# Softmax maxima and inverse sums spread by DMA, scores half a tile further ahead, one output bank per MLP, weight setup reordered

## The reference

```
kv_flat = mean over 4x4 windows of kv, @ w_sr        # 768 keys, k = v
s = (q @ k.T) / sqrt(128);  s = s - s.max(-1)
a = exp(s);  a /= a.sum(-1) + 1e-9;  x = a @ v
h = x @ w_in1;  y = (max(h, 0) + alpha * min(h, 0)) @ w_out1      # 2048 hidden features
h = y @ w_in2;  out = (h * sigmoid(1.702 h)) @ w_out2
```

## Time and profile before

| | us |
|---|---|
| median of 3 runs | 1409.24 (1408.22 to 1411.01) |
| span of the profiled execution | 1407.1 |
| TensorE busy | 1365.1 (97%) |
| VectorE busy | 1088.8 (77%) |
| ScalarE busy | 823.9 (59%) |
| GpSimd busy | 444.9 (32%) |

### The profile page before, as it was taken

One profiled execution on the slowest core, in us unless ns is written; L12 is line 12 of the kernel. 1 busy time (PEld: TensorE's weight loads), 2 busy tenths in 40 slices (PEclk: granted clock), 3 DMA queues, 4 the chain that ended last, 5 costly groups with the idle time before them and its releaser, 6 DMA issues.

```text
span 1407.1 us, 19487 instructions
## 1 busy us (share of the span) xinstructions
PE 1365.1 (97%) x6000; PEld 1094.6 (78%) x6000; DVE 1088.8 (77%) x1689; ACT 823.9 (59%) x1417; POOL 444.9 (32%) x295
## 2 busy tenths in 40 slices
PE   4599999999999999999999999999999999999998
PEld 3477887887887878878878788788787787887776
DVE  6868878778678787787786887877968877778775
ACT  2465665656656656656566566565665665655644
POOL 2740522413405314234054142241440522413400
PEclk8699999999999999999999999999999999999999
DMA  7100000000000000000000000000000000000000
GB/s 255 68 1 16 0 15 15 0 15 7 7 15 7 7 15 0 15 7 7 15 7 7 15 0 15 15 0 15 7 7 15 0 15 15 0 15 0 8 8 8
DMA packets 9514, 23.26 MB, mean 17 GB/s; under 512 B 1184, under 2 KB 1312, under 8 KB 8992
## 3 DMA queue, kind: packets, MB, share of 16 engines
q1 hardware_dynamic: 6048, 16.85, 3.6%
q10 hardware_dynamic: 3456, 6.29, 1.2%
HBM read 16.85 MB, written 6.29 MB: 16 GB/s over the span
## 4 chain that ended last, share of the span: by engine, by line
PE 90%; DVE 6%; ACT 1%; DMA 1%; issue 0%; SPq 0%; DVEq 0%; ACTq 0%
PE ps_y L639 14%; PE ps_y L641 13%; PE ps_y L640 13%; PE ps_h L641 12%; PE ps_h L639 12%; PE ps_h L640 12%; PE ps_s L639 4%; PE ps_s L640 4%; PE ps_s L641 4%; DVE g_lo L545 3%; PE ps_t L670 2%; PE ps_t L682 2%; DMA kv_raw<-kvT 1%; ACT g_full L372 1%; DVE g_hi L543 1%; DVE wide L502 0%
## 5 line engine op out<-in xcount | busy, mean ns | idle before, releaser
L283 POOL TENSOR_TENSOR s_sb<-s_sb,max_sb 128x512 f32<-128x512 f32 x138 | 205.3, 1523 | 577.6 <-ACT max_sb L349 577.6
L537 DVE SCALAR_TENSOR_TENSOR g_lo<-ps_h,g_hi 128x512 fp32r<-128x512 f32 x384 | 264.0, 688 | 153.1 <-ACT g_hi L367 150.5
L372 ACT ACTIVATE g_full<-ps_h 128x512 f32<-128x512 f32 x384 | 229.8, 598 | 252.6 <-PE ps_h L641 247.6
L545 DVE TENSOR_TENSOR g_lo<-g_full,g_hi 128x512 fp32r<-128x512 f32 x384 | 309.6, 806 | 13.1
L639 PE MATMUL ps_y<-g_hi,down_hi 128*128 128x512 f32 x768 | 313.4, 408 | 1.6 <-DVE g_lo L545 0.5
L641 PE MATMUL ps_y<-g_hi,down_lo 128*128 128x512 f32 x768 | 303.4, 395 | 0.0
L640 PE MATMUL ps_y<-g_lo,down_hi 128*128 128x512 f32 x768 | 302.4, 394 | 0.0
L367 ACT ACTIVATE g_hi<-ps_h 128x512 fp32r<-128x512 f32 x384 | 229.1, 597 | 94.2 <-PE ps_h L641 81.7
L543 DVE CAST g_hi<-g_full 128x512 fp32r<-128x512 f32 x384 | 161.9, 422 | 28.1 <-ACT g_full L372 28.0
L639 PEld LDWEIGHTS ps_y<-g_hi,down_hi 128*128 128x128 f32 x768 | 144.7, 188 | 47.7 <-DVE g_lo L545 18.6
L515 DVE TENSOR_TENSOR a_lo<-s_sb,a_hi 128x512 fp32r<-128x512 f32 x144 | 171.3, 1190 | 1.2 <-ACT a_hi L362 1.2
(11 more groups left out here) (90 smaller groups left out, 1774.9 us busy)
## 6 DMA issues: line engine op xcount, KB each, us to landing
kv_raw<-kvT SPq DMA_DIRECT2D x12, 512.0 KB, 5.4
q_raw<-qT SPq DMA_DIRECT2D x24, 256.0 KB, 2.6
outT<-out_sb ACTq DMA_DIRECT2D x24, 256.0 KB, 2.0
w_raw<-w_in SPq DMA_DIRECT2D x2, 1024.0 KB, 6.2
w_raw<-w_out SPq DMA_DIRECT2D x2, 1024.0 KB, 7.3
wsr_sb<-w_sr SPq DMA_DIRECT2D x1, 64.0 KB, 3.2
alpha_sb<-alpha SPq DMA_DIRECT2D x1, 8.0 KB, 3.5
```

What stands on the lines that cost most here:

```text
L283: nc.gpsimd.tensor_tensor(s_sb[:, c, :], s_sb[:, c, :], max_sb[:], ALU.subtract).then_inc(diff_done, 1)
L372: nc.scalar.activation(g_full[:, f % RING, :], ps_h[:, f % RING, :], ACT.Gelu_apprx_sigmoid).then_inc(act_done, 1)
L537: nc.vector.scalar_tensor_tensor(g_lo[:, f % RING, :], ps_h[:, f % RING, :], 0.0, f32(g_hi[:, f % RING, :]), ALU.max, ALU.subtract).then_i ...
L545: nc.vector.tensor_tensor(g_lo[:, f % RING, :], g_full[:, f % RING, :], f32(g_hi[:, f % RING, :]), ALU.subtract).then_inc(g_split, 1)
```

## The change

The maxima and the inverse sums no longer go through `wide`, four transposes and a PSUM bank. SP stores the 128x4 column to a row of 512 values in the chip's memory and loads that row back to all 128 partitions (`spread_max`, `spread_inverse`). The bank `ps_t` goes, and so does one bank of `ps_s`, which now takes scores and turned columns by turns; `ps_x` holds the attended values, which VectorE reads there directly; `ps_y1` and `ps_y2` hold the outputs of the two MLPs. Scores, maxima and queries now belong to tile t + 2: scores in the GELU half, queries in the relu half. Eight of the 16 GELU casts go to ScalarE, the output store goes from ScalarE to SP, and a tiny GELU loads ScalarE's table ahead of the copy of y. Ahead of the loop w_in1 comes already turned, the second MLP's weights have a place of their own and are split in pieces of 512 columns, and the scores of tile 1 are made there.

The diff, cut to its core (constants, banks, SP, GpSimd, ScalarE, VectorE, TensorE; `spread_inverse` is made as `spread_max`, and waits for the division before it instead of the subtraction):

```diff
+    EXP_AT = {7: 0, 9: 1, 10: 2, 12: 3, 13: 4, 15: 5}
+    LO_AT = {8: 0, 10: 1, 11: 2, 13: 3, 14: 4}
+    ATTEND_AT = {11: 0, 13: 1, 14: 2}
+    QUERIES_AT = 5
+    SUMS_AT = LAG
+    SCORES_AT = {5: 0, 7: 1, 8: 2, 10: 3, 12: 4, 13: 5}
+    DIVIDE_AT = 9
+    CAST_ON_ACT = (1, 3, 5, 7, 9, 11, 13, 15)
+    max_row = nc.dram_tensor("max_row", (BLOCKS, P), F32, kind="Internal").ap()
+    inv_row = nc.dram_tensor("inv_row", (BLOCKS, P), F32, kind="Internal").ap()
...
-        ps_s = psum("ps_s", [P, 2, 512])
-        ps_t = psum("ps_t", [P, 512])
-        ps_y = psum("ps_y", [P, 512])
+        ps_x = psum("ps_x", [P, 512])
+        ps_s = psum("ps_s", [P, 512])
+        ps_y1 = psum("ps_y1", [P, 512])
+        ps_y2 = psum("ps_y2", [P, 512])
...
+            def spread_max(u):
+                sp.wait_ge(col_max_done, u + 1)
+                with nc.allow_non_contiguous_dma(reason="a column of 512 values"):
+                    sp.dma_start(max_row.rearrange("b p -> p b"), col_max[:]).then_inc(max_stored, DMA)
+                if not first(u):
+                    sp.wait_ge(diff_done, u * KC)
+                sp.wait_ge(max_stored, u * DMA + DMA)
+                row = max_row.rearrange("b p -> (b p)").rearrange("(o n) -> o n", o=1)
+                sp.dma_start(max_sb[:], row.broadcast_to([P, TOK])).then_inc(max_in, DMA)
...
+            load_queries(1)
+            spread_max(0)
+            load_queries(2)
+            spread_inverse(0)
+            spread_max(1)
+            with sp.Fori(0, TILES - 3) as t:
+                load_queries(t + 3)
+                spread_inverse(t + 1)
+                spread_max(t + 2)
+                store(t)
...
-            with pool.Fori(1, TILES - 1) as u:
-                subtract_max(u)
-                sum_exponentials(u)
-                queries_lo(u + 1)
+            for m, (hi, lo) in enumerate(((up_hi[1], up_lo[1]), (down_hi[1], down_lo[1]))):
+                for i in range(PIECES):
+                    pool.wait_ge(w2_hi, m * PIECES + i + 1)
+                    nc.gpsimd.tensor_tensor(lo[:, piece(i)], w_raw2[:, m * FF + i * PIECE:m * FF + (i + 1) * PIECE],
+                                            f32(hi[:, piece(i)]), ALU.subtract).then_inc(w2_lo, 1)
+            with pool.Fori(0, TILES - 2) as t:
+                queries_lo(t + 2)
+                subtract_max(t + 1)
+                sum_exponentials(t + 1)
...
+                if f in CAST_ON_ACT:
+                    act.wait_ge(act_done, t * UPS + (CH + f + 1))
+                    nc.scalar.copy(g_hi[:, f % RING, :], g_full[:, f % RING, :]).then_inc(act_cast, 1)
...
+            def tile(t, attend, score):
                 for f in range(LAG, CH):
...
+                    relu_hi(t, f)
+                    if attend and f in EXP_AT:
                         exponentials(t + 1, EXP_AT[f])
...
                         exponentials_hi(t + 1, EXP_AT[f])
...
+                nc.scalar.activation(warm_out[:], warm[:], ACT.Gelu_apprx_sigmoid)
...
+                    if score and f in SCORES_AT:
+                        scores_to_sbuf(t + 2, SCORES_AT[f])
...
+            act.dma_start(w_in1T_sb, w_in1T).then_inc(w_in[2], DMA)
             scores_to_sbuf(0, KC - 1)
+            act.wait_ge(pooled_made, KV_CHUNKS)
+            act.dma_start(w_raw2[:, 0:FF], w_in2).then_inc(w_in[3], DMA)
+            act.dma_start(w_raw2[:, FF:2 * FF], w_out2).then_inc(w_in[4], DMA)
...
+            for c in range(KC):
+                scores_to_sbuf(1, c)
+            act.wait_ge(w_in[3], DMA)
+            for i in range(PIECES):
+                nc.scalar.copy(up_hi[1][:, piece(i)], w_raw2[:, i * PIECE:(i + 1) * PIECE]).then_inc(w2_hi, 1)
             attended_hi(0)
...
-                dve.wait_ge(x_raw_made, u + 1)
-                dve.wait_ge(inv_spread, u + 1)
-                nc.vector.tensor_tensor(x_full[:], x_full[:], ps_t[:], ALU.mult).then_inc(x_made, 1)
...
+            def tile(t, attend, score):
                 for f in range(LAG, CH):
...
                     relu_lo(t, f)
...
+                    if score and f == QUERIES_AT:
+                        queries_hi(t + 2)
+                    if attend and f in LO_AT:
+                        weights_lo(t + 1, LO_AT[f])
+                for c in range(len(LO_AT), KC if attend else 0):
+                    weights_lo(t + 1, c)
                 dve.wait_ge(y_hi_made, t + 1)
...
+                nc.vector.tensor_tensor(y_lo[:], ps_y1[:], f32(y_hi[:]), ALU.subtract).then_inc(y_split, 1)
                 for f in range(CH):
                     gelu_parts(t, f)
...
+                    if attend and f == SUMS_AT:
                         inverse_sums(t + 1)
...
+                    if score and SCORES_AT.get(f, 0) >= 1:
+                        chunk_max(t + 2, SCORES_AT[f])
+                    if attend and f == DIVIDE_AT - 1:
                         divide(t + 1)
...
+                    if attend and f == DIVIDE_AT:
                         attended_lo(t + 1)
...
+                if attend:
                     for f in range(LAG):
                         relu_lo(t + 1, f)
+                        if score and f == 1:
+                            token_max(t + 2)
...
+                elif c == 0:
+                    pe.wait_ge(col_sum_done, u)
+                else:
+                    pe.wait_ge(scores_out, u * KC + c)
...
+            def tile(t, attend_next, score):
                 for f in range(LAG, CH):
                     up(t, 0, f)
...
                     down(t, 0, f - LAG)
...
+                    if attend_next and f in ATTEND_AT:
                         attend(t + 1, ATTEND_AT[f])
...
+                passes(ps_y1[:], mix_hi[:], mix_lo[:], x_hi[:], x_lo[:], False, False)
                 for f in range(CH - LAG, CH):
                     down(t, 0, f)
...
+                for c in range(len(ATTEND_AT), KC if attend_next else 0):
+                    attend(t + 1, c)
+                if first(t):
+                    pe.wait_ge(w2_lo, 2 * PIECES)
                 for f in range(CH):
                     up(t, 1, f)
...
+                    if attend_next and f == SUMS_AT:
                         turn_sums(t + 1)
...
+                    if score and f in SCORES_AT:
+                        scores(t + 2, SCORES_AT[f])
                     if f >= LAG:
                         down(t, 1, f - LAG)
                 for f in range(LAG):
...
+                    if attend_next:
                         up(t + 1, 0, f)
+                        if score and f == 1:
+                            turn_max(t + 2)
                     down(t, 1, CH - LAG + f)
...
+            turn_sums(0)
+            for c in range(KC):
+                scores(1, c)
             pe.wait_ge(up0_lo_made, 1)
             for f in range(LAG):
                 up(0, 0, f)
+                if f == 1:
+                    turn_max(1)
```

More of the change, by code:

```diff
@@ L22 @@
 DMA = 16
+PIECE = 512
 def attention_mlp_kernel(
@@ L208, in cols, with piece, score_bank, casts_before @@
             return slice(b * P, (b + 1) * P)
+        def piece(i):
+            return slice(i * PIECE, (i + 1) * PIECE)
         def first(t):
             return isinstance(t, int) and t == 0
[L213 to L220, removed]
+        def score_bank(u, c):
+            return ps_x[:] if first(u) and c % 2 == 0 else ps_s[:]
+        mix_ps = ps_y1[:, 0:C]
+        CASTS_ACT = len(CAST_ON_ACT)
+        CASTS_DVE = CH - CASTS_ACT
+        def casts_before(f, on_act):
+            return sum((j in CAST_ON_ACT) == on_act for j in range(f))
         block = ctx.enter_context(nc.Block())
@@ L242, in _ @@
             sp.dma_start(w_raw[1][:], w_out1).then_inc(w_in[1], DMA)
[L244 to L258, removed]
+            load_queries(1)
[8 more added lines that the diff above has]
+                store(t)
+            spread_inverse(TILES - 2)
+            spread_max(TILES - 1)
+            store(TILES - 3)
+            spread_inverse(TILES - 1)
+            store(TILES - 2)
+            store(TILES - 1)
+            sp.wait_ge(out_stored, DMA * TILES)
         @block.gpsimd
@@ L575, in tile @@
                         inverse_sums(t + 1)
-                    if not last and f == SPREAD_SUMS_AT:
+                    if score and SCORES_AT.get(f, 0) >= 1:
+                        chunk_max(t + 2, SCORES_AT[f])
+                    if attend and f == DIVIDE_AT - 1:
                         divide(t + 1)
-                    if not last and f == SPREAD_SUMS_AT + 1:
+                    if attend and f == DIVIDE_AT:
                         attended_lo(t + 1)
-                    if prepare and f == CH // 2:
-                        queries_hi(t + 2)
@@ L582, in tile @@
-                if not last:
+                if attend:
                     for f in range(LAG):
                         relu_lo(t + 1, f)
+                        if score and f == 1:
+                            token_max(t + 2)
             per_chunk = KV_CHUNKS // KC
```

(15 more changed lines are left out.)

289 lines of the change are left out of this document (107 added, 182 removed).

## The result

The kernel after takes **1712.92 us** (median of 4 runs, 1710.02 to 1715.44) against 1408.95 of the kernel before, run beside it: ratio **1.2151, 95% interval 1.2133 to 1.217**. The prediction said 1381, within 1374 to 1403. The miss is 332 us.

The account below looks back on a forecast made before the run. TensorE, busy 97% of the span, was taken to bound the kernel. Terms -20.2 (transposes), -10.9 (gaps), -4.2 (scores leaving the loop), +5 (preamble) and +1 (small waits) gave -29 us: 1381 us, within 1374 to 1403.

Parts of the forecast that it names:

- the price of the trip: Column stored by SP and loaded as a row to 128 partitions: 5.4 us, of which store 2.6; maxima hidden up to 7.5.
- the late row: Rival: the row of maxima comes too late, costing 22 x (R - 7.5) for a trip of R us; chance 0.12.
- The second trip: Inverse sums in the GELU half: row at 9.3 us, division at about 11.5, about 3 us of room behind; costs nothing.
- the break-even: Before attend(0): GpSimd waits for the maxima past a 6.9 us trip; TensorE loses time one for one past 7.5 us.
- the tile: Steady tile of the loop: 54.4 to 54.6 us, against 55.84 before.
- a set of transposes: Four transposes on TensorE cost 0.44 us; removing two sets in each of 23 tiles gains 20.2 us.
- the table load that hides: ScalarE's 1.28 us load ends about 0.4 us before y is complete; rival that it does not hide: +12 us, chance 0.06.
- one bank: One bank for scores and turned sums adds no wait; rival of 0.3 us a tile, +7 us, chance 0.14.
- the maxima of tile 1 behind x_lo: At the start, the third up waits some 2 us for these maxima, giving an effective start of 76.5.
- The preamble: Ahead of the loop: first up at 74.5, loss of 5 us (bounds +2 and +9); rival +9 more, chance 0.08.
- the gaps: Two TensorE gaps a tile, 0.32 and 0.16 us, from slow VectorE subtractions beside GpSimd; ending both gains 10.9 us.

Follow-up runs that it names:

- the kernel with 16 byte runs: The kernel after, with each transpose taking every fourth token, so a store writes 128 runs of 16 bytes instead of 512 of 4: 1390.76 us, ratio 0.9865.
- one extra load: Against the 16 byte layout, SP loads the row of maxima once more to an unused place and waits for it before the load that counts: 1446.21 us.

## Why the prediction was wrong

**The step that failed** is the price of the trip, the 5.4 us that it was given. It was bounded by the two nearest rows, a 256 KB store and the small `alpha` load: 2.0 to 3.5 us for the store, 2.6 for the load. Neither row writes runs of four bytes, and the text said so ("no row prices 512 descriptors of 4 bytes"), yet it took the quiet end and gave the late row a chance of 0.12. The store took 8.6, the load 5.1, the trip 13.7. `alpha` is a load, and 64 bytes in one run a partition; the column is four runs of 4 bytes. The rows had transfers that were near in size or quick, none near in form, and the form decided.

**Mis-sized behind it**: a late microsecond. The rival priced it one for one behind 7.5 us. At a trip of 13.7 us that gives 22 x 6.2 = 136 us for the maxima alone, 1517; the kernel with that trip alone took 1571. Of the 54 us between them the loop has 35 (62.3 us a tile instead of 60.7) and the start with tile 0 nearly all of the rest (the first up at 84.92, the copy of y 38.61 us later). In the loop the idle time was even priced too high, 5.2 us instead of 6.2, since the trip there is 13.2 us and the break-even 8.1; what the rival left out is the lower clock behind the stall, by which TensorE is busy for 2.4 us a tile more than the 54.72 of the kernel with 16 byte runs, and for 4.0 more where there are two stalls (means of the loop's tiles: 57.1 and 58.8). **The second trip** was set at nothing, rightly at 5.4 us; VectorE was at the division 7.9 us after its store (617.12, from 609.25), so at 13.3 us it cost a stall of 3.3.

**Right mechanism, wrong place**: the break-even was worked out for attend(0). GpSimd was free 6.7 us after the store (forecast 6.9), and attend(0) waits from a trip of 7.4 us on (forecast 7.5). But at the long trip it isn't an attend that waits. ScalarE's exponential holds the relu behind it, and TensorE waits, from 8.1 us on, for a down product of the tile at hand. With one extra load the waits are shared between the two.

**Right**: the tile, 54.60 and 54.72 us (forecast 54.4 to 54.6, so the second is 0.1 over); a set of transposes, 0.45 us (20.6 by 46; forecast 0.44); the table load that hides; one bank, with a small margin (0.4 us forecast; with the queries put back the reduction came about 1.3 us later, and TensorE lost 1.15); the maxima of tile 1 behind x_lo (a wait of 2.06 us; forecast 2). With the trip at 5.5 us the kernel takes 1390.8: inside the forecast's range, 10 us above its point.

**The preamble** has most of those 10 us. The copy of y of tile 0 comes at 110.57, 9.4 us later than before (101.12), where the sum had about 1 (5, less the 4.2 of the scores that go). Half of that is the first up, at 79.22 instead of 74.5. The order of ScalarE's queue was in the sum (six chunks of scores, four casts, then x_hi and x_lo), and the subtractions began 3.8 us later than before, within the bounds of 1.8 and 4.8. But the inverse was ready at 61.8 instead of 59.6, and a chunk took 2.32 us, the upper end of the 1.6 to 2.3 that it was given. That is the granted clock. In the execution profiled with the transposes made twice a chunk took 1.64 us, and the first up started at 74.91. The stretch from 60 to 70 us of both, the kernel with 16 byte runs first:

```profile
60.00:70.00 10.00, 7.02 (x15) 3.55 (x14) 5.41 (x8) 1.75 (x3) 0.00 (x0) 0.50 0.15 28
60.00:70.00 10.00, 5.67 (x20) 2.87 (x19) 5.49 (x8) 2.93 (x5) 0.00 (x0) 0.97 0.12 28
```

What set the clock there isn't shown. The rest, some 4 us, lies in tile 0, where the clock is 0.58 from 80 to 90 us and was 1.00 before. What the sum took as given is the queue's order: x_full was ready at 69.8, but its copy stood behind three copies of scores and four casts until 77.4. With it ahead of them the first up starts at 74.01, and the time is 1385.14.

**Half right**: the gaps. 55.84 less 54.60 is 1.24 us a tile, 0.88 of it transposes, 0.36 of the 0.48 that the gaps were worth. Where they went was read wrongly for the second of them: moving the queries isn't what ends it, since with the queries back the kernel is as fast once the sums have their own bank. That the freed VectorE has the room is the likely reason; it wasn't tried by itself.

## What to carry to other kernels

Price a transfer by the form of its runs, not by its bytes: if no row has the form, time it alone before it goes on a path with a fixed deadline, or lay the data out so that a partition's values are neighbours in memory. Give an inserted wait a deadline, and look at what stands behind the waiting instruction on each engine down the line; here the first victim was an unrelated relu. Price a stall of TensorE above its own length, and try the clock's share out: here TensorE's busy time of a tile grew by 0.5 us behind most stalls of 1.4 to 2.1 us, and by 2.4 to 4.0 in the mean behind those of 4 us and more.

## What the runs showed of the hardware

- 512 floats from 128 partitions to memory: 8.2 to 9.3 us as runs of 4 bytes, 1.4 to 2.4 as 128 runs of 16, 1.13 to 1.15 as one run from one partition. The Trainium skill (DMA: Bandwidth & Descriptors, "Specifications") has read-modify-write for what is under 512 bytes; the rows agree for the 4 byte runs in that they are slow, but the 16 byte runs, under the same bound, are 3.5 to 6.6 times quicker, round by round.
- One 2 KB row read to 128 partitions takes 3.0 to 3.7 us alone (up to 5.0 behind the 4 byte store) and 4.1 in the kernel with 16 byte runs; 128 different rows take 2.64 alone.
- TensorE stood from 649.6 to 655.3. Its granted clock was 1.00 from 650 to 652, 0.80 from 652 to 654, 0.50 from 654 to 660, and 0.99 from 660 to 661. Idle times of 1.4 to 2.1 us in a tile left the tile's mean clock at 1.00 in 15 of 22 tiles and at 0.97 in 7.
- Ahead of the loop, six chunks of scores in the same order ran at a clock of 0.50 in one execution (2.32 us each) and of 0.97 in another (1.64 us each).
